# Attention and two MLPs on one core: the first two heads of the attention in another order on all engines

## The reference

```python
q_assign = argmax(q_n @ c_n.T); k_assign = argmax(k_n @ c_n.T)    # 16 clusters per head
scores = where(q_assign == k_assign, (q @ k.T) / sqrt(64), -1e9)   # 2 x 8 heads, 768 x 768
attn = exp(scores - rowmax(scores)); attn = attn / (rowsum(attn) + 1e-9)
x = (attn @ v), heads side by side                                 # 1536 tokens x 512
h = x @ w_in;  g = max(h, 0) + alpha * min(h, 0);   x = g @ w_out   # 512 -> 2048 -> 512
h = x @ w_in2; g = P(h) / (Q(|h|) + 1e-6);          out = g @ w_out2
```

## Time and profile before

| | |
|---|---|
| median of 3 runs | 805.09 us (804.35 to 805.61) |
| the profiled execution | 805.12 us, span 803.3 us |
| PE busy | 786.7 us (98%), 4339 matmuls |
| DVE, ACT, POOL busy | 558.6, 486.3, 292.5 us |
| end of the attention's PE work | about 260 us |

### The profile page before, as it was taken

The page is one execution under the profiler, slowest core; times in us unless marked ns, Lnnn a source line. Parts: engine busy times, 40 slices in busy tenths (PEclk is TensorE's granted clock), DMA queues, the critical chain, the costliest instruction groups (busy, mean ns, idle before and its releaser), DMA issues.

```text
span 803.3 us, 13103 instructions
## 1 busy us (share of the span) xinstructions
PE 786.7 (98%) x4339; PEld 747.2 (93%) x4339; DVE 558.6 (70%) x950; ACT 486.3 (61%) x836; POOL 292.5 (36%) x328
## 2 busy tenths in 40 slices
PE   6999999999999999999999999999999999999997
PEld 5789999999999999999999999999888988998896
DVE  5777877877875555544454354478898888888886
ACT  2467777877788111211211143388999999999996
POOL 7466987988984698000000037640000000000000
PEclk9999999999999999999999999999999999999999
DMA  7445664564432233000000025410001001001001
GB/s 198 125 113 148 156 160 117 152 163 125 120 103 73 92 96 96 1 0 0 0 0 0 0 67 157 123 49 1 1 0 39 0 0 39 0 0 40 1 0 40
DMA packets 30316, 52.15 MB, mean 65 GB/s; under 512 B 9184, under 2 KB 11328, under 8 KB 30272
## 3 DMA queue, kind: packets, MB, share of 16 engines
q1 hardware_dynamic: 30272, 51.59, 23.5%
HBM read 29.40 MB, written 3.19 MB: 41 GB/s over the span
## 4 chain that ended last, share of the span: by engine, by line
PE 82%; DVE 7%; ACT 6%; issue 2%; POOL 1%; DMA 1%; SPq 0%; ACTq 0%; DVEq 0%; POOLq 0%
PE ps L206 27%; PE ps L1017 15%; PE ps L1028 12%; PE ps L647 5%; PE ps L678 4%; PE ps L689 4%; PE ps L708 4%; PE ps L709 4%; PE ps L716 4%; PE ps L622 3%; ACT scratch L1095 1%; DVE g_f L1179 1%; DVE corr L1166 1%; ACT scratch L1093 1%; DVE scratch L1175 1%
## 5 line engine op out<-in xcount | busy, mean ns | idle before, releaser
L212 ACT ACTIVATE g_hi<-g_f 128x384 fp32r<-128x384 f32 x128 | 67.3, 526 | 216.4 <-PE ps L1017 193.2
L216 DVE TENSOR_TENSOR g_lo<-g_f,g_hi 128x384 fp32r<-128x384 f32 x128 | 78.5, 613 | 82.7 <-ACT g_hi L212 82.7
L206 PE MATMUL ps<-x_hi,w_hi_b 128*128 (+1 forms) x352 | 118.8, 337 | 0.5 <-POOL w_lo_b L1198 0.5
L206 PE MATMUL ps<-x_hi,w_lo_b 128*128 (+1 forms) x352 | 118.7, 337 | 0.0
L206 PE MATMUL ps<-x_lo,w_hi_b 128*128 (+1 forms) x352 | 118.7, 337 | 0.0
L796 ACT ACTIVATE probs_hi<-ps 128x768 fp32r<-128x768 f32 x96 | 78.1, 814 | 58.2 <-PE ps L689 57.4
L905 DVE TENSOR_REDUCE row_max<-ps 128x1 fp32r<-128x768 f32 x96 | 90.9, 950 | 32.0 <-PE ps L647 31.7
L355 DVE TENSOR_TENSOR probs_lo<-ps,probs_hi 128x768 fp32r<-128x768 f32 x66 | 62.9, 953 | 21.9 <-ACT ps L799 21.9
L224 DVE TENSOR_SCALAR corr<-ps,alpha_c 128x384 f32<-128x384 f32 x64 | 39.4, 616 | 46.5 <-PE ps L206 46.3
L1198 POOL TENSOR_TENSOR w_lo_a<-stage,w_hi_a 128x512 fp32r<-128x512 f32 x10 | 13.3, 1355 | 157.2 <-ACT w_hi_a L1115 157.2
L206 PEld LDWEIGHTS ps<-x_hi,w_hi_b 128*128 128x128 f32 x352 | 66.1, 188 | 2.7 <-issue 0.8
(11 more groups left out here) (132 smaller groups left out, 2088.9 us busy)
## 6 DMA issues: line engine op xcount, KB each, us to landing
stage<-in_moe_w_in SPq DMA_DIRECT2D x27, 256.0 KB, 2.6
stage<-in_moe_w_out SPq DMA_DIRECT2D x27, 256.0 KB, 2.8
raw<-in_qk SPq DMA_DIRECT2D x16, 384.0 KB, 4.2
op_a<-head_hi SPq DMA_DIRECT2D x32, 192.0 KB, 3.4
v_raw<-in_v SPq DMA_DIRECT2D x16, 192.0 KB, 2.5
op_b<-head_hi SPq DMA_DIRECT2D x16, 192.0 KB, 3.4
op_b<-head_lo SPq DMA_DIRECT2D x16, 192.0 KB, 3.6
scratch<-spread SPq DMA_DIRECT2D x16, 192.0 KB, 4.7
```

The costliest lines, as they stand in the source:

```text
L206: last = pe.matmul(h_ps[j % H_RING][:, 0:BLK], a[:, 0, w], x[:, kt, cols], start=(kt == 0 and i == 0), stop=(kt == KT - 1 and i == 2))
L212: act.activation(g_hi[:, j % 2], g_f[:, j % 2], ACT.Copy).then_inc(g_hi_made, 1)
L216: dve.tensor_tensor(g_lo[:, j % 2], g_f[:, j % 2], g_hi[:, j % 2].bitcast(F32), ALU.subtract)\
```

## The change

For heads 0 and 1 the loops of PE, DVE, POOL and SP are replaced by lists of calls (`WRITTEN_OUT = 2`; the loops go on with head 2, turn g = 12).

- `turn_first_max(t)` turns one tile's maximum as a matmul to a row of bank 4, partition 0. ACT writes the negative of the row of 384 straight into `op_b`, without a DMA.
- The maxima of heads 0 to 3 are handed over by halves of three tiles (for head 0 only the second is left): `turn_max(m, h)`, `take_max(m, h)`, `put_max(m, h)`. The first half is needed by unit 0, the second by unit 3.
- Guards come when they are needed. Three fewer are done by turn 12 (18 for 21), and heads 2 and 3 do seven and eight each.
- `score` may be split into `score_a` and `score_b`. `sim(2)` goes from ahead of the first score to behind it.
- POOL makes the rests of units 0, 2, 3 and 5 of head 0. From head 1 on the division is as before.
- `put_mask_q` of heads 1 to 3 goes from DVE to ACT (`put_mask_q_early`), where it and `put_mask_k` stand ahead of exp(2), exp(6) and exp(10).
- At the start, the copies to `cent_t` go ahead of the table load on ACT and ahead of `head_lo` on DVE.

```diff
-        POOL_LO = (0, 3)
+        POOL_LO = {0: (0, 2, 3, 5), N - 1: ()}
...
+            def first_max(t0, t1):
+                return ps[0:1, 4, t0 * P:t1 * P]
+            GUARD = {(2, 0): {2: (3, 0)}, (2, 1): {2: (3, 1)}, (2, 2): {3: (3, 2)}, (2, 3): {2: (3, 3), 3: (3, 4)},
+                     (2, 4): {2: (3, 5)}, (2, 5): {2: (4, 0)}, (3, 0): {1: (4, 1), 3: (4, 2)}, (3, 1): {2: (4, 3)},
+                     (3, 2): {3: (4, 4)}, (3, 3): {2: (4, 5)}, (3, 4): {2: (5, 0), 3: (5, 1)}, (3, 5): {2: (5, 2)}}
+            TURNED = {(2, 0): (2, 1), (2, 3): (3, 0), (2, 5): (3, 1), (3, 4): (4, None)}
+            WRITTEN_OUT = 2
...
 # SP, behind load_qk(3)
-                (three tiles' maxima to op_b), put_max(0), load_v(1), load_w(0), ...; for n in range(N): ...
+                load_v(1); load_w(0); load_w(1) ...; put_max(0, 1); copy_a(2); copy_b(2); load_qk(4)
+                put_max(1, 0); copy_a(3); copy_b(3); put_max(1, 1); load_v(2); load_w(2); load_qk(5)
+                move_sums(0); put_max(2, 0); load_v(3); load_w(3); for n in range(WRITTEN_OUT, N): ...
 # POOL, behind split_v(0)
+                split_head(2); make_lo(0); split_head(3); make_lo(2); make_lo(3); mark_nearest(2)
+                split_v(1); make_lo(5); split_w(0); make_lo(6); split_v(2); split_head_hi(4)
+                mark_nearest(3); make_lo(9); split_head_lo(4); mark_nearest(4); split_w(1)
 # PE
-                    at_least(pe, guard_taken, T * m + t - (1 if m == 0 else 0))
+                    at_least(pe, guard_taken, T * m + t - (1 if m == 0 and t < T - 1 else 0))
...
+                def turn_first_max(t):
+                    pe.wait_ge(guard_taken, t + 1)
+                    made = pe.matmul(first_max(t, t + 1), row_max[:, t:t + 1], ident_r[:], start=True, stop=True)
...
+                guard(0, 0..2); turn_first_max(0); guard(0, 3); turn_first_max(1); turn_first_max(2)
+                score(0); guard(0, 4); score(1); weigh_hi(0); guard(0, 5); score(2); turn_onehot(1)
+                turn_max(0, 1); weigh_hi(1); weigh_lo(0); score_a(3); weigh_lo(1); guard(1, 0); sim(2)
+                guard(1, 1); score_b(3); weigh_hi(2); guard(1, 2); score(4); weigh_lo(2); turn_max(1, 0)
+                guard(1, 3); weigh_hi(3); score(5); weigh_lo(3); guard(1, 4); weigh_hi(4); turn_onehot(2)
+                score(6); weigh_lo(4); guard(1, 5); weigh_hi(5); score(7); weigh_lo(5); turn_max(1, 1)
+                guard(2, 0); guard(2, 1); weigh_hi(6); score(8); sim(3); weigh_lo(6); weigh_hi(7)
+                guard(2, 2); score(9); weigh_lo(7); turn_max(2, 0); guard(2, 3); weigh_hi(8)
+                turn_onehot(3); score(10); sim(4); weigh_lo(8); weigh_hi(9); guard(2, 4); score(11)
+                weigh_lo(9); guard(2, 5); for g in range(WRITTEN_OUT * U, UNITS + LAG): ...
 # ACT
-                act.preload_act_table_set("natural_log_exp_and_others")    (ahead of the cent_t copy)
+                act.preload_act_table_set("natural_log_exp_and_others")    (behind it)
-                act.activation(neg_max[0:FIRST_T], max_at(0, FIRST_T), ACT.Copy, scale=-1.0).then_inc(max_taken, 1)
-                (wait for the DMA, then the same for all six tiles)
+                act.activation(op_b[96:97, 0, Q_SIDE, 0:HS], first_max(0, FIRST_T), ACT.Copy, scale=-1.0)\
+                   .then_inc(first_max_put, 1)
                 for g in range(UNITS):
+                    if g in (2, 6, 10):
+                        put_mask_k((g + 2) // 4)
+                        put_mask_q_early((g + 2) // 4)
                     exp(g)
 # DVE, behind put_mask_q(0)
+                take_guard(0, 0..3); nearest(1); ranked(1); take_guard(0, 4); first_nearest(1)
+                mark_nearest(1); take_guard(0, 5); take_max(0, 1); make_lo(1); take_guard(1, 0)
+                nearest(2); take_guard(1, 1); ranked(2); first_nearest(2); take_guard(1, 2); take_max(1, 0)
+                take_guard(1, 3); make_lo(4); take_guard(1, 4); take_guard(1, 5); take_max(1, 1)
+                take_guard(2, 0); make_lo(7); take_guard(2, 1); nearest(3); make_lo(8); take_guard(2, 2)
+                ranked(3); first_nearest(3); take_max(2, 0); take_guard(2, 3); nearest(4); make_lo(10)
+                ranked(4); first_nearest(4); take_guard(2, 4); make_lo(11); take_guard(2, 5)
```

More of the change, by code:

```diff
@@ L288, in guard_at @@
             def guard_at(m, t):
-                b = 5 if m == 0 and t % 2 else 0
+                b = 5 if m == 0 and t in (1, 3) else 0
                 return ps[:, b:b + 2, 0:HS]
-            SIM_BANK = {1: 7, 2: 4}
+            SIM_BANK = {1: 7, 2: 7}
             def sim_at(m, t):
@@ L456, in _ @@
                 sp.dma_start(coef[:, 4:6], coef_b.partition_broadcast(P)).then_inc(const_loaded, 16)
-                for n in range(N):
+                put_max(0, 1)
+                copy_a(2)
+                copy_b(2)
+                load_qk(4)
+                put_max(1, 0)
+                copy_a(3)
+                copy_b(3)
+                put_max(1, 1)
+                load_v(2)
+                load_w(2)
+                load_qk(5)
+                move_sums(0)
+                put_max(2, 0)
+                load_v(3)
+                load_w(3)
+                for n in range(WRITTEN_OUT, N):
+                    if n == 2:
+                        put_max(2, 1)
                     if n + 2 < N:
@@ L691, in score, with s_half @@
                     last.then_inc(s_made, 1)
+                def s_half(n, u):
+                    if n < HALVED:
+                        return {0: 0, TH: 1}.get(u)
+                    return 1 if u == 0 else None
+                def score(g):
+                    score_a(g)
+                    score_b(g)
                 def weigh_hi(g):
@@ L739, in _ @@
                 guard(0, 1)
-                sim(2, range(0, 2))
                 guard(0, 2)
+                turn_first_max(0)
                 guard(0, 3)
-                sim(2, range(2, 3))
-                turn_first_max()
+                turn_first_max(1)
+                turn_first_max(2)
+                score(0)
                 guard(0, 4)
+                score(1)
+                weigh_hi(0)
                 guard(0, 5)
-                sim(2, range(3, 5))
-                turn_max(0)
@@ L749, in _ @@
-                for g in range(UNITS + LAG):
+                score(2)
+                turn_onehot(1)
+                turn_max(0, 1)
+                weigh_hi(1)
+                weigh_lo(0)
+                score_a(3)
+                weigh_lo(1)
+                guard(1, 0)
+                sim(2)
+                guard(1, 1)
+                score_b(3)
+                weigh_hi(2)
+                guard(1, 2)
+                score(4)
+                weigh_lo(2)
+                turn_max(1, 0)
@@ new lines, in _ @@
+                guard(1, 3)
+                weigh_hi(3)
+                score(5)
+                weigh_lo(3)
+                guard(1, 4)
+                weigh_hi(4)
+                turn_onehot(2)
+                score(6)
+                weigh_lo(4)
+                guard(1, 5)
+                weigh_hi(5)
+                score(7)
+                weigh_lo(5)
+                turn_max(1, 1)
+                guard(2, 0)
+                guard(2, 1)
+                weigh_hi(6)
+                score(8)
@@ new lines, in _ @@
+                sim(3)
+                weigh_lo(6)
+                weigh_hi(7)
+                guard(2, 2)
+                score(9)
+                weigh_lo(7)
+                turn_max(2, 0)
+                guard(2, 3)
+                weigh_hi(8)
+                turn_onehot(3)
+                score(10)
+                sim(4)
+                weigh_lo(8)
+                weigh_hi(9)
+                guard(2, 4)
+                score(11)
+                weigh_lo(9)
+                guard(2, 5)
@@ L750, in _ @@
+                for g in range(WRITTEN_OUT * U, UNITS + LAG):
                     n, s = g // U, g % U
-                    if g >= LAG:
-                        weigh_hi(g - LAG)
+                    weigh_hi(g - LAG)
                     if g < UNITS:
-                        if g == U - 2:
-                            sim(3)
-                        if g == U - 1:
-                            turn_max(1)
-                        if s == 0 and n >= 1 and n + 2 < N:
+                        if s == turn_pair(n) and n + 2 < N:
@@ L931, in _ @@
                 put_mask_q(0)
-                for t in range(T):
+                for t in range(FIRST_T + 1):
                     take_guard(0, t)
```

256 lines of the change are left out of this document (157 added, 99 removed).

## The result

The changed kernel takes **812.78 us** (median of 6 runs, 811.42 to 814.53), the kernel before 805.15 on the same chip (6 runs, 804.35 to 805.85). The ratio is 1.0096, with an interval of 1.0082 to 1.0111: 7.6 us slower, where 802.6 and a gain of 2.5 were predicted. The profiled execution took 812.46.

The account below looks back on a forecast made before the run. PE, busy 98% of the span, was taken as the bound. Turn 12 3.9 us earlier, less 1.1, 0.2 and 0.1 behind it, left 2.5: 805.12 - 2.5 = 802.6, range 801.3 to 803.9 (8 in 10: 800.5 to 805.4).

Parts of the forecast that it names:

- Start and first score: Kernel start: sim(0) at 5.92, 0.98 us earlier; first guard at 13.43; first score at 17.5, 4.8 us earlier.
- Level of PE: Heads 0 and 1: PE rises to 2.4 GHz at 22.8, after 16 matmuls; the other 120 go at 0.18 us.
- rival (b): Heads 0 and 1: PE's level rises earlier, at 20.9, or the waits overlap; 801.6 us, chance 0.18.
- Waits up to turn 12: PE's waits at guards, sims, transposes and maxima before turn 12 sum to 5.3 us; turn 12 starts at 54.9.
- What is hidden: Masks on ACT, rests on POOL, SP's DMAs and DVE's extra reductions (87% busy in heads 2 and 3) stay behind PE.
- three guards more (1.1), a wait of 0.2, two turns of maxima (0.1): Behind turn 12: what is left to do there, taken off the 3.9 us gained before it, leaving 2.5 us.
- Its own sign of being wrong: Attention: among the signs that the prediction is wrong, heads 2 and 3 taking more than 14.69 + 0.7 us each.
- Rival (e): Slower: ACT's masks ahead of exp(2), exp(6) and exp(10) make PE wait, 3 x 1.6 = 4.8; 807.4 us, chance 0.10.
- Rival (d): Attention: POOL's rests hold DVE 1.24 us each, two ahead of a guard's reduction; 805.1 us, chance 0.08.
- The rule quoted in the prediction: A DVE instruction with two SBUF inputs and a GpSimd instruction reading SBUF exclude each other for their whole length.
- Rival (c): Heads 0 and 1: PE's level rises late, at about 30; 2.8 us lost, 805.4 us, chance 0.11.

Follow-up runs that it names:

- mask first: Changed kernel with DVE's put_mask_q(4) ahead of guard (3, 1)'s reduction and nearest(5): 807.68 us, 1.0035.
- wait filled: Changed kernel with 14 matmuls, whose result is overwritten, ahead of weigh_hi(12): 809.6 us, 1.0063.
- shorter wait: Changed kernel with DVE's put_mask_q(4) between guard (3, 1)'s reduction and nearest(5): 809.8 us, 1.0059.
- the fault in the kernel before: Kernel before with head 4's transposes and masks in turn 13 instead of turn 12: 808.48 us, 1.0044.
- `return 0`: Changed kernel with the transposes and masks of head 4 back in turn 12: 806.45 us, 1.0013.

## Why the prediction was wrong, by its own steps

- **Start and first score: right.** sim(0) at 6.02 (5.92), the first guard at 13.25 (13.43), the first score at 17.40 (17.5). ACT's row of 384 ran at 17.64 and took 0.48.
- **Level of PE: wrong in place by some 3.5 us, and worth nothing.** I placed the rise at 22.8, behind 16 matmuls; the pairs at 19.42 and 19.77 already start 0.35 apart. That is 12 matmuls at 0.18 instead of 0.32, 1.7 us, more than the 1.0 of rival (b), but PE then waits for DVE at `turn_onehot(1)` and the gain is gone. The versions with the same start show it: the level rises 1.6 us behind the first score in the changed kernel (17.40 and 19.04) and 4.5 us behind it in the one with both masks of head 4 on ACT (17.37 and 21.89), and yet in all eleven traces with this start the transposes begin 5.99 to 6.01 us behind the first score. In the latter PE doesn't wait for them at all:

```profile
21.57 0.52 PE L806 MATMUL ps<-probs_hi,v_hi 128*128 128x384 f32 x1
21.89 0.39 PE L807 MATMUL ps<-probs_hi,v_lo 128*128 128x384 f32 x1
...
23.38 0.52 PE L712 MATMUL ps<-ident_b,onehot 128*64 128x128 bf16 x6
```

So the list of instructions alone didn't settle the place of the rise, and here it didn't matter. Rival (b), with 801.6, is wrong for this reason too.
- **Waits up to turn 12: the sum 5.3, measured 4.6, but not the same ones.** Guards (2, 1) and (2, 5) waited 1.34 and 0.92 (1.5 and 1.35), turn_onehot(3) 0.59 (0.7). At turn_onehot(1) I took nothing and it waited 1.25; score_a(3) had 0.5 and no idle time stands ahead of it. That turn 12 came at 55.06 against 54.9 is partly luck, in two places. Up to `turn_onehot(1)` (23.39, by my walk 23.5) the earlier level and the wait that I had at nothing cancel. From there to turn 12 it took 31.7 us for my 31.4, but with waits of 3.4 for 5.2, while the 116 matmuls of 384 columns took 22.9 besides for 20.9: they lose about 0.1 behind each sim and each set of transposes, and some behind each wait. The profile's idle time is also shorter than what a wait costs: from 21.62 to 23.39 PE lost 1.77 less the 0.35 of two matmuls, 1.4, for a wait of 1.25.
- **"What is hidden" and the line "three guards more (1.1), a wait of 0.2, two turns of maxima (0.1)": this step failed.** The prediction followed the lists to turn 12 and put everything behind it down as full rate. It argued heads 2 and 3 by DVE's share (87%, "still below PE"), which is no argument: the longest wait comes from the order within a turn. Its own sign of being wrong, heads 2 and 3 of more than 14.69 + 0.7, is what came (head 3 took 18.1). Instead of 1.4 us, 11.6 were lost from turn 12 to the MLPs: the late mask 5.1 (2.54 idle and 2.6 of low rate), the waits at the doubled guards 3.1 (0.97, 0.78, 0.33, 0.98), the 1.4 that were counted, 0.5 behind head 3, and about 1.5 for what each wait costs beside its idle time and small gaps. The first is shown by four kernels (mask first, wait filled, shorter wait, and the fault in the kernel before), the second by the version without any guard to catch up, whose heads 2 and 3 ran without a wait. That it is the doubling which costs isn't shown: one by one the same three guards made PE wait as well. `turn_pair` in the loops of PE, DVE and ACT gave the place of the first, and I never walked it.
- **Rival (e), "slower: the masks ahead of the exps come into the open"**, had the sign, and its 4.8 us for masks is near the 5.1 of this place, but its time of 807.4 is 5.4 short, and it had the wrong masks. The ones of heads 1 to 3, moved to ACT, never made PE wait; the one of head 4, left on DVE, did.
- **Rival (d), POOL's rests hold DVE:** up to turn 12 one hold, of 1.7 us, and it was where I counted "about 1 us". DVE's and POOL's timelines in the changed kernel:

```profile
10.29 0.36 DVE L399 TENSOR_TENSOR from_first<-first_rank,rank 128x192 bf16<-128x192 bf16 x1
...
20.87 2.03 DVE L399 TENSOR_TENSOR from_first<-first_rank,rank 128x192 bf16<-128x192 bf16 x1
```

```profile
20.85 1.83 POOL L390 TENSOR_TENSOR probs_lo<-probs,probs_hi 128x768 fp32r<-128x768 f32 x1 [2.12 <-ACT probs L943]
```

The same instruction took 0.36 us free and 2.03 beside the rest, and it is what turn_onehot(1) waits for. The rule quoted in the prediction (the Trainium skill, SBUF — State Buffer, Who interferes with whom) agrees: the hold lasts for POOL's whole instruction. With the level as late as I had placed it, the hold would have cost nothing, as I wrote; with the earlier level it is what takes the gain, by the timelines (no kernel leaves it out). But it is by rest 0, which POOL makes in the kernel before too. The two rests that the change moves to POOL held nothing, and moving them back cost 2.8 us, part of it by a hold of its own. So as a rival (d) is wrong.
- **Rival (c)**, the level late, did not occur at the start, but a lower level did occur, behind the 2.54 us wait.

**What stays open.** Behind head 3 the better versions lose another 0.6 to 1.6 us. In the one with `return 0` two waits stand there (178.49 and 238.88 above). Waits of both kinds are in the trace of the kernel before with only its start changed too (0.39 at 176.94, 0.73 at 237.34), so it isn't shown that they come from the change, and what makes them come in one trace and not in another is open. Ahead of the first, ACT works on `rows` and `scratch` only when the head's sums have come back by DMA. Such a DMA, at about 230 us, took 2.8 us to land in the kernel before, 4.3 with `return 0` and 4.2 (at 236.9) in the changed kernel. But of those between 100 and 226 us, where this wait lies, the medians are 2.9, 2.9 and 2.2, so the traces don't bear it out as the cause, and no kernel tests it.

## What to carry to other kernels

When the head of a pipeline is rewritten, walk every list at least two turns past the seam, above all the steps that are moved by a turn there, and ask of each which instruction of its engine's list now stands ahead of it. Work that is put off ("three guards fewer by turn 12") is not saved: it needs a place where the other engines have room, and the busy share of a head doesn't say whether there is one. A wait on a full PE may cost twice its length, once as idle time and once as the lower rate behind it, so the longest wait is the one to remove first. And what PE gains ahead of a step that waits for another engine is not gained: look for the next such step before pricing it.

## What the runs showed of the hardware

- Of three waits of PE at the same place of its list, one trace each, 0.48 and 1.88 us of idle time left the starts 0.18 us apart; 2.54 us brought them to 0.32 (granted clock 0.51, the level of 1.2 GHz). In the changed kernel that was at once and for 18 matmuls, in the kernel before with the late mask some 1.5 us after the wait and for about 11. Filled with 14 useless matmuls, the same time left the level alone.
- At the start of both kernels the granted clock reads 1.00 while matmuls start 0.32 to 0.4 us apart; behind the wait at 64.59 it reads 0.51 for the same distance. So at the start the level is read from the starts.
- With one and the same list of instructions PE's starts went from 0.32 to 0.18 us apart at different places in different traces: 1.6 us behind the first score in the changed kernel, 4.5 us behind it in the version with both masks on ACT.
- A DVE instruction with two bf16 inputs in SBUF took 0.36 us free and 2.03 beside a subtraction of POOL (20.85 to 22.68, changed kernel), another 0.25 free and 1.92 beside one (30.65 to 32.47, two rests back on DVE). Each ended less than 0.3 us behind POOL's.
